# The prologue of an attention kernel with two MLPs shared out anew between the engines

## The reference

```
q, k, v: (4, 8, 768, 64)   mem_k, mem_v: (4, 8, 8, 64)   fp32
for each chunk of 32 queries:
    keys   = 8 memory keys + 16 to the left + the chunk + 8 to the right (clipped at the ends)
    scores = q_c @ keys.T / 8 ;  scores -= max(scores)
    a = exp(scores);  a /= sum(a) + 1e-9
    out_c = a @ values
x = out as (3072 tokens, 512)
h = x @ w_in (512 x 2048);  g = max(h, 0) + alpha * min(h, 0);  y = g @ w_out (2048 x 512)
z = (y @ w_a) * (y @ w_b) (512 x 1536);  result = z @ w_out2 (1536 x 512)
```

## Time and profile before

| | |
|---|---|
| median of 3 runs | 1223.64 us (1218.63, 1223.64, 1223.72) |
| profiled execution | 1219.24 us, span 1217.4 us |
| TensorE busy | 1205.3 us, 6634 matmuls |
| VectorE busy | 783.9 us (64%) |
| ScalarE busy | 571.8 us (47%) |
| GpSimd busy | 248.7 us (20%) |
| DMA | 87.84 MB, 72 GB/s on the mean |
| granted TensorE clock | 1.00 |

### The profile page before, as it was taken

One profiled execution on the slowest core, in us unless ns is written; L12 is line 12 of the kernel. 1 busy time (PEld: TensorE's weight loads), 2 busy tenths in 40 slices (PEclk: granted clock), 3 DMA queues, 4 the chain that ended last, 5 costly groups with the idle time before them and its releaser, 6 DMA issues.

```text
span 1217.4 us, 19013 instructions
## 1 busy us (share of the span) xinstructions
PE 1205.3 (99%) x6634; PEld 1095.9 (90%) x6637; DVE 783.9 (64%) x1452; ACT 571.8 (47%) x1412; POOL 248.7 (20%) x226
## 2 busy tenths in 40 slices
PE   8899999999999999999999999999999999999998
PEld 5799999999999999999999888888888888888887
DVE  7788777777777777777656466854376644465421
ACT  6765545454545455454323455543444443444322
POOL 1687323332323232323025100000000000000000
PEclk9999999999999999999999999999999999999999
DMA  6453212212112121121021411022102021111000
GB/s 268 134 154 112 85 60 72 71 58 84 58 58 84 58 84 58 58 85 40 5 92 35 160 74 70 36 96 69 44 35 70 35 97 68 44 36 69 1 36 34
DMA packets 27612, 87.84 MB, mean 72 GB/s; under 512 B 2720, under 2 KB 6816, under 8 KB 25248
## 3 DMA queue, kind: packets, MB, share of 16 engines
q1 hardware_dynamic: 23328, 80.76, 19.7%
q10 hardware_dynamic: 4224, 6.29, 1.4%
HBM read 74.46 MB, written 12.58 MB: 71 GB/s over the span
## 4 chain that ended last, share of the span: by engine, by line
PE 95%; DVE 3%; ACT 1%; issue 1%; POOL 0%; ACTq 0%; DVEq 0%; POOLq 0%
PE bank L570 15%; PE bank L572 15%; PE bank L571 15%; PE bank L578 9%; PE bank L577 9%; PE bank L576 9%; PE bank L813 5%; PE bank L814 5%; PE bank L812 5%; PE bank L620 2%; PE bank L589 1%; PE bank L588 1%; PE bank L595 1%; DVE g_lo L1206 0%; PE bank L605 0%
## 5 line engine op out<-in xcount | busy, mean ns | idle before, releaser
L577 PE MATMUL bank<-yc,ws 128*128 128x512 f32 x504 | 196.1, 389 | 0.0
L578 PE MATMUL bank<-yc,ws 128*128 128x512 f32 x504 | 196.1, 389 | 0.0
L576 PE MATMUL bank<-yc,ws 128*128 128x512 f32 x504 | 196.1, 389 | 0.0
L1196 DVE TENSOR_SCALAR g_neg<-bank,al 128x384 f32<-128x384 f32 x128 | 79.0, 617 | 121.2 <-PE bank L572 121.2
L883 ACT ACTIVATE prob<-prob,neg_max 96x128 f32<-96x128 f32 x220 | 85.7, 391 | 110.5 <-DVE neg_max L1161 110.5
L577 PEld LDWEIGHTS bank<-yc,ws 128*128 128x128 f32 x504 | 94.6, 188 | 19.7
L578 PEld LDWEIGHTS bank<-yc,ws 128*128 128x128 f32 x504 | 94.6, 188 | 19.6
L576 PEld LDWEIGHTS bank<-yc,ws 128*128 128x128 f32 x504 | 94.6, 188 | 19.6
L1392 DVE TENSOR_TENSOR p_split<-p_all,p_split 128x512 fp32r<-128x512 f32 x72 | 49.5, 691 | 93.5 <-ACT p_split L1078 93.4
L912 ACT ACTIVATE g_hi<-g_raw 128x384 fp32r<-128x384 f32 x128 | 67.1, 525 | 86.7 <-DVE g_raw L1201 84.1
L1078 ACT ACTIVATE p_split<-p_all 128x512 fp32r<-128x512 f32 x72 | 45.2, 631 | 110.3 <-PE bank L814 100.8
(11 more groups left out here) (150 smaller groups left out, 3036.8 us busy)
## 6 DMA issues: line engine op xcount, KB each, us to landing
u_raw<-units SPq DMA_DIRECT2D x53, 576.0 KB, 3.7
wr<-w_ab SPq DMA_DIRECT2D x18, 1024.0 KB, 4.8
u_early<-units SPq DMA_DIRECT2D x11, 576.0 KB, 8.8
y_dram<-y_stage ACTq DMA_DIRECT2D x8, 768.0 KB, 3.9
out<-o_stage SPq DMA_DIRECT2D x24, 256.0 KB, 2.0
w_raw<-w SPq DMA_DIRECT2D x16, 256.0 KB, 3.3
y_stage<-w SPq DMA_DIRECT2D x16, 256.0 KB, 3.0
wr<-y_dram SPq DMA_DIRECT2D x8, 512.0 KB, 4.4
```

Source lines behind the costliest of these rows:

```text
L576: nc.tensor.matmul(out_ap, w_hi, m_hi, start=first, stop=False, skip_group_check=True)
L577: nc.tensor.matmul(out_ap, w_hi, m_lo, start=False, stop=False, skip_group_check=True)
L578: return nc.tensor.matmul(out_ap, w_lo, m_hi, start=False, stop=True, skip_group_check=True)
L1196: nc.vector.tensor_scalar(g_neg[:, :], h_ps[:, 0:TOK], 0.0, al[:, j:j + 1], ALU.min, ALU.mult)\
```

## The change

In the prologue and in the tiles, `softmax_max` becomes four `tensor_tensor_reduce` operations per unit (one for each block): the sum of scores and mask, times -1/8 (or -1/16, see below), with the minimum of the result written out as the negated maximum; the exponential then has the scale -1. TensorE's next score waits for all four. `score_early` multiplies all 128 rows, in which k and q stand twice, so that early scores are twice as large and their scale is halved. The 1e-9 is added by a reduction over the sum and a constant beside it instead of by an operation with a scalar.

In the prologue GpSimd normalises instead of VectorE, and VectorE copies the transposes instead of ScalarE. The halves of a pair (mix, x_hi, x_lo) alternate, one for each unit, and unit 8's softmax stands in the loop with the others. The early weight pieces, v and k/q splits are placed anew. The fillers read a constant of ones that the program has anyway; there are ten ahead of the first score instead of eight, four to two for the first units, none for units 3 to 7 and fewer around tile 0. The last pair's mix is put one part of `up` later, `lo_g` of the first chunk ahead of the softmax. VectorE's loop over t = 1 to 5 is written out, since the mask of a block is now picked by a number.

```diff
+        def inverses(b):
+            return inv_sum[:, b].rearrange("p (b o) -> p b o", o=1).to_broadcast([QB, BLOCKS, KEYS])
+
+        def score_scale(u):
+
+            return -SCALE / 2 if u <= HEADS else -SCALE
...
         def w_in_prologue(u):
-            return {1: (0,), 2: (1,), 6: (2,), 8: (3,)}.get(u, ())
+            return {0: (0,), 2: (1,), 5: (2,), 8: (3,)}.get(u, ())
...
-            for n in range(W_PROLOGUE):
-                lo_w(n)
-            lo_v(HEADS, HEADS)
-            lo_unit(HEADS + 1, HEADS + 1)
+            def normalise(u):
+                buf = prob_early[u % 2]
+                pool.wait_ge(inv_done, u + 1)
+                nc.gpsimd.tensor_tensor(buf[:, :, :], buf[:, :, :], inverses(u % 2), ALU.mult).then_inc(prob_done, 1)
+
+            for u in range(HEADS + 1):
+                normalise(u)
+                for n in w_in_prologue(u):
+                    lo_w(n)
+                if u == 4:
+                    lo_v(HEADS, HEADS)
+                if u == 6:
+                    lo_v(HEADS + 1, HEADS + 1)
+            pool.wait_ge(w_lo_done, W_PROLOGUE)
+            pool.wait_ge(v_lo_done, 2)
+            lo_kq(HEADS + 1, HEADS + 1)
...
                 if not isinstance(u, int) or u >= 1:
-                    pe.wait_ge(mask_added, u)
+                    pe.wait_ge(neg_done, u)
...
             def keep_busy(n):
 
+                ones = nc.const_aps.tensor(1.0, [P, 512], mybir.dt.bfloat16)
                 for i in range(n):
-                    nc.tensor.matmul(o_ps[:, :], filler[:, 0:P], filler[:, P:], start=True, stop=True)
+                    nc.tensor.matmul(o_ps[:, :], ones[:, 0:P], ones, start=True, stop=True)
 
             def score_early(u):
 
                 pe.wait_ge(early_loaded[u], 16)
                 if u:
-                    pe.wait_ge(mask_added, u)
+                    pe.wait_ge(neg_done, u)
                 for i in range(BLOCKS):
-                    q = u_early[0:HEAD_DIM, u, Q0 + i * QB:Q0 + (i + 1) * QB]
+                    q = u_early[:, u, Q0 + i * QB:Q0 + (i + 1) * QB]
                     at = slice(i * KEYS, (i + 1) * KEYS)
-                    last = nc.tensor.matmul(s_ps[0:QB, at], q, u_early[0:HEAD_DIM, u, at], start=True, stop=True)
+                    last = nc.tensor.matmul(s_ps[0:QB, at], q, u_early[:, u, at], start=True, stop=True)
...
                 for kt in range(KT):
-                    if first_tile and j == 0 and kt == 1:
-
+                    if first_tile and j == 0 and kt == 2:
+                        keep_busy(2)
                         mix_early(PAIRS - 1, 0)
                         mix_early(PAIRS - 1, 1)
...
-                            if first and j == 1:
-                                keep_busy(3)
...
                             if first and p == 0:
-                                keep_busy(4)
+                                keep_busy(2)
...
-            pe.wait_ge(filler_ready, 1)
-            keep_busy(8)
+            keep_busy(10)
             score_early(0)
             for u in range(HEADS + 1):
-                keep_busy(3)
+                if u < 3:
+                    keep_busy(4 - u)
                 if u < HEADS:
                     score_early(u + 1)
-                if u >= 3 and u % 2:
-                    mix_early(u // 2 - 1, 0)
-                    mix_early(u // 2 - 1, 1)
-                if u in (1, 2, HEADS):
-                    keep_busy(3)
                 if u == 1:
                     pe.wait_ge(consts, 1)
                 if u:
-                    transpose_probs(u - 1, u % 2 == 1)
+                    if u < 3 or u == HEADS:
+                        keep_busy(3)
+                    transpose_probs(u - 1, False)
+                if u >= 3 and u // 2 <= PAIRS:
+
+                    mix_early((u - 3) // 2, (u - 3) % 2)
...
                     last = nc.scalar.activation(dst[:, i, :], src[:, i, :], ACT.Exp,
-                                                bias=neg_max[:, b, i:i + 1], scale=SCALE,
-                                                accum_out=row_sum[:, b, i:i + 1])
+                                                bias=neg_max[:, b, i:i + 1], scale=-1.0,
+                                                accum_out=row_sum[:, b, i, 0:1])
...
-            def copy_pt(u):
-
-                act.wait_ge(transposed, u + 1)
+            for u in range(HEADS + 1):
+                exps(u, u % 2, masked_early[u % 2], prob_early[u % 2])
                 if u >= 4:
-                    act.wait_ge(mixed, u - u % 2 - 2)
-                nc.scalar.activation(pt_early[:, (u // 2) % 2, :, u % 2, :],
-                                     pt_ps[:, 0:TOK].rearrange("p (b q) -> p b q", b=BLOCKS),
-                                     ACT.Copy).then_inc(pt_copied, 1)
-
-
-            for u in range(HEADS):
-                exps(u, u % 2, masked_early[u % 2], prob_early[u % 2])
-                if u >= 3 and u % 2:
-                    split_x(u // 2 - 1, 0, u // 2 - 1, 0, True)
-                    split_x(u // 2 - 1, 1, u // 2 - 1, 0, True)
-                if u:
-                    copy_pt(u - 1)
+                    split_x((u - 4) // 2, u % 2, (u - 4) // 2, 0, True)
                 for n in w_in_prologue(u):
                     hi_w(n)
+                if u == 3:
+                    hi_v(HEADS, HEADS)
                 if u == 5:
-                    hi_v(HEADS, HEADS)
-                if u == 6:
                     hi_v(HEADS + 1, HEADS + 1)
-            copy_pt(HEADS - 1)
-            for n in w_in_prologue(HEADS):
-                hi_w(n)
-            hi_kq(HEADS + 1, HEADS + 1, 0)
+                if u == 7:
+                    hi_kq(HEADS + 1, HEADS + 1, 0)
+            split_x(PAIRS - 2, 1, PAIRS - 2, 0, True)
             split_x(PAIRS - 1, 0, PAIRS - 1, 0, True)
             split_x(PAIRS - 1, 1, PAIRS - 1, 0, True)
-            exps(HEADS, 0, masked_early[0], prob_early[0])
...
-                nc.vector.tensor_tensor(dst[:, :, :], s_ps[0:QB, :].rearrange("p (b k) -> p b k", b=BLOCKS),
-                                        mask[:, bass.ds(half, BLOCKS), :], ALU.add).then_inc(mask_added, 1)
-                dve.wait_ge(mask_added, u + 1)
-                nc.vector.tensor_reduce(row_max[:, b], dst[:, :, :], AX_X, ALU.max).then_inc(max_done, 1)
-                dve.wait_ge(max_done, u + 1)
-                nc.vector.tensor_scalar(neg_max[:, b], row_max[:, b], -SCALE, None, ALU.mult)\
-                    .then_inc(neg_done, 1)
-
-            def normalise(u, b, buf=prob):
+
+                for i in range(BLOCKS):
+                    last = nc.vector.tensor_tensor_reduce(
+                        out=dst[:, i, :], in0=s_ps[0:QB, i * KEYS:(i + 1) * KEYS], in1=mask[:, half + i, :],
+                        scale=score_scale(u), scalar=FAR, op0=ALU.add, op1=ALU.min, accum_out=neg_max[:, b, i:i + 1])
+                last.then_inc(neg_done, 1)
+
+            def invert_sums(u, b):
                 dve.wait_ge(exp_done, u + 1)
-                nc.vector.tensor_scalar(row_max[:, b], row_sum[:, b], 1e-9, None, ALU.add).then_inc(sum_done, 1)
+                nc.vector.tensor_reduce(row_total[:, b], row_sum[:, b], AX_X, ALU.add).then_inc(sum_done, 1)
                 dve.wait_ge(sum_done, u + 1)
-                nc.vector.reciprocal(inv_sum[:, :], row_max[:, b]).then_inc(inv_done, 1)
+                if isinstance(u, int) and u >= 2:
+                    dve.wait_ge(prob_done, u - 1)
+                nc.vector.reciprocal(inv_sum[:, b], row_total[:, b]).then_inc(inv_done, 1)
+
+            def normalise(u, b):
+                invert_sums(u, b)
                 dve.wait_ge(inv_done, u + 1)
-                nc.vector.tensor_tensor(buf[:, :, :], buf[:, :, :],
-                                        inv_sum[:, :].rearrange("p (b o) -> p b o", o=1)
-                                        .to_broadcast([QB, BLOCKS, KEYS]),
-                                        ALU.mult).then_inc(prob_done, 1)
+                nc.vector.tensor_tensor(prob[:, :, :], prob[:, :, :], inverses(b), ALU.mult).then_inc(prob_done, 1)
+
+            def copy_pt(u):
+                dve.wait_ge(transposed, u + 1)
+                if u >= 4:
+                    dve.wait_ge(mixed, u - u % 2 - 2)
+                nc.vector.tensor_copy(pt_early[:, (u // 2) % 2, :, u % 2, :],
+                                      pt_ps[:, 0:TOK].rearrange("p (b q) -> p b q", b=BLOCKS)).then_inc(pt_copied, 1)
...
                     bend(t, 4 * p, first)
                     if attention:
                         split_pt(g * 2, 0)
+                    if first and p == 0:
+                        lo_g(t, 0)
+                    if attention:
                         softmax_max(g * 2 + 1, 1, half, prob)
-                    lo_g(t, 4 * p)
+                    if not (first and p == 0):
+                        lo_g(t, 4 * p)
                     if p == 0 and not first:
...
+            nc.vector.memset(row_sum[:, :, :, 1], 1e-9)
...
```

(27 more changed lines are left out.)

16 lines of the change are left out of this document (5 added, 11 removed).

## The result

The changed kernel takes 1212.75 us (median of five runs, 1212.38 to 1214.58) against 1219.34 for the kernel before, run beside it (five runs, 1218.63 to 1223.72): a ratio of 0.9937 with an interval of 0.9914 to 0.996. The direction held, and 1212.75 lies in the range, 0.75 us from its lower end. The size didn't hold: profiled execution against profiled execution the forecast was 3.9 us, and it is 6.9 (1212.38 against 1219.24; spans 1210.6 and 1217.4). Nor did the likeliest outcome: I gave 0.57 to a change of under 6.1 us and 0.35 to a larger gain, and the medians are 6.6 us apart.

A forecast was written before the change was run, and what follows sets the result against it. TensorE was taken to bound the kernel, with VectorE setting T8 in the prologue. Gains of 0.6 + 0.2 + 1.3 + 1.8 = 3.9 us took the median of 1223.64 to 1219.7 us, range 1212 to 1226.

The forecast's parts named there:

- The price s: VectorE time of a unit's four fused softmax operations: 1.5 us, between 1.2 and 1.95, in place of 1.54.
- high bound: Each fused softmax operation pays an accumulator read as long as ScalarE's, 0.19 us, which makes s 1.95 us.
- T8: Time when TensorE begins unit 8's transposes: 40.0 us against 40.62, 0.6 gained, with ends of +3.3 and -3.4.
- formula: Prologue: first softmax at 6.8, five periods of s + 1.2, three of s + 1.7, then the tail: T8 = 26.5 + 9s.
- the units are in before they are needed: Prologue DMAs keep their order, and 418 GB/s from 10 to 20 us fall to 58 after 30, so data comes in time.
- The start: Before the first score: an earlier filler start can bring the clock up sooner, 0 to 0.65 us, 0.2 taken.
- Pair 1: Fillers ahead of TensorE's wait for g_lo go and g_lo moves ahead of the softmax: 1.3 us gained.
- Pairs 3 and 4: The sum on VectorE, now a reduction, takes 0.17 instead of 1.07 us: 0.9 off each pair, 1.8 together.
- A: Rival: fused operation cheap (s = 1.2), tile 0 gets back what it can; 7.1 to 9.3 us gained, 1214.3 to 1216.5; chance 0.28.
- B: Rival: fused operation pays its accumulator read in full (s = 1.95); 3.4 lost, 3.3 gained, 1223.7 us; chance 0.20.
- C: Rival: with fewer prologue fillers TensorE's clock falls; 9.8 us lost, 3.7 gained, 1229.7; chance 0.10.
- D: Rival: busy GpSimd hands the gain back as waits for weights; about 1 us gained, 1222.6; chance 0.07.

The follow-up runs named there:

- e10_two_moved: The changed kernel with two ScalarE steps one unit later, the high part of v of unit 8 and the third weight piece: 1210.75 us.
- e12_last_weight_later: `e10_two_moved` with the fourth weight piece split later, behind the last x_hi on ScalarE and behind lo_kq of unit 9 on GpSimd: 1209.56 us.
- e2_fused_one_by_one: The changed kernel with a wait between the four fused softmax operations of a unit, so each starts when the one before has ended: 1212.29 us.
- e6_g_lo_behind: The changed kernel with g_lo of the first chunk behind the softmax again: 1212.48 us.
- e1_three_ops: The changed kernel with the softmax as three operations again (mask added, maximum, negated maximum), in prologue and tiles: 1216.63 us.
- f1_fused_alone: The kernel before with only the four fused softmax operations, TensorE's wait for them and VectorE's loop written out: 1214.99 us.
- e7_scalar_sum: The changed kernel with the sum of a unit in the tiles as an operation with a scalar again instead of a reduction: 1214.20 us.

## Why the prediction was right or wrong, step by step

**The price s: the step that failed.** I had 1.5 between 1.2 and 1.95; it is 0.93. The length was right (0.283 for 0.29), the distance between starts was not: I took it to be the length, a small gap and 0.08 for the read of the accumulator, 0.38 in all, and it is 0.213. The high bound, an accumulator read paid in full, fell as well: the read takes 0.08 and lies under the next operation. One of my two rows, the x_lo pieces of the earlier trace rows, does start as far apart as it is long (0.36 and 0.352). Another row of the same trace showed that this isn't general:

```profile
10.68 0.69 DVE L1170 TENSOR_TENSOR prob<-prob,inv_sum 96x512 f32<-96x512 f32 x1
11.29 0.68 DVE L1156 TENSOR_TENSOR y_stage<-bank,mask 96x512 f32<-96x512 f32 x1
```

The second starts 0.61 us after the first, which is 0.69 long. The x_lo pieces alternate between the lower and the upper 64 partitions; these two and the fused operations all start at partition 0. The Trainium skill (VectorE: DVE Perf Modes, Two Vector instructions with no wait between them) says that an instruction is held until the earlier ones end when an input or its output starts in another quadrant than the last one read from, or written to, the same memory. The spacings, 0.21 for the ones and 0.36 for the others, agree with it; no run here changed the quadrants alone, so that the form of the operations makes the difference isn't excluded. The Trainium skill (VectorE: DVE Perf Modes, The DRAIN you can't avoid) tells of chained copies that took the same time with and without waits, and adds that an operation that isn't held starts earlier. Here it does: 0.21 apart without a wait, 0.33 with one. The mere number of operations, which had spoken for the high bound, does not decide here: four fused ones take 0.93 us where three took 1.54.

I also priced the negated maximum of the kernel before at the 0.17 of an undisturbed stretch. In its prologue it takes 0.353 on the mean:

```profile
L1161 DVE TENSOR_SCALAR neg_max<-row_max 96x4 f32<-96x4 f32 x9 | 3.2, 353 | 0.3
```

**T8.** The formula's sum comes close where ScalarE waits for no DMA (33.9 and 33.8 for the measured 34.24 and 33.80 of `e10_two_moved` and `e12_last_weight_later`), but in part by luck. In `e10_two_moved` the first five periods take 11.5 us instead of 5(s + 1.2) = 10.7, the next three 7.0 instead of 3(s + 1.7) = 7.9, and the tail 9.05 instead of 8.6. VectorE's period from unit 5 on is s + 1.4, because the reciprocal and the copy too are overlapped by what follows them:

```profile
19.58 0.29 DVE L1157 CUSTOM_DVE_ANT_0 y_stage<-bank,mask 96x128 f32<-96x128 f32 x1
...
20.43 0.15 DVE L1164 TENSOR_REDUCE row_total<-row_sum 96x4 f32<-96x8 f32 x1
20.62 0.17 DVE L1168 RECIPROCAL inv_sum<-row_total 96x4 f32<-96x4 f32 x1
20.71 0.54 DVE L1179 COPY pt_early<-bank 128x384 f32<-128x384 f32 x1
21.17 0.71 DVE L1193 TENSOR_TENSOR x_lo<-bank,x_hi 64x192 fp32r<-64x192 f32 x2
21.91 0.29 DVE L1157 CUSTOM_DVE_ANT_0 y_stage<-bank,mask 96x128 f32<-96x128 f32 x1
```

In `e2_fused_one_by_one`, with s = 1.28, the formula gives 37.9 and is 0.9 too high. ScalarE's 2.2 us a unit left out what else it does: with `hi_v` (0.40), a weight piece (0.63) or `hi_kq` (0.95) between, its exponentials of units 5 to 8 start 2.7, 2.9 and 3.2 us apart in `e10_two_moved`. The changed kernel falls short of the formula by 2.0 us, and the sentence that failed there is that the units are in before they are needed. I checked that against the mean bandwidth of the kernel before and not against the new place of `hi_v(8)`: two units earlier in a faster loop, it came up at 15.9 us and its data at 18.05. In the kernel before it ran at 25.51, without a wait. Which share the new place has and which the faster loop wasn't taken apart; with the two steps moved T8 comes 2.35 us earlier. That GpSimd takes 1.3 for the normalisation was too much (1.03), the copy's length of 0.55 right (0.534), the score of full height as assumed 1.08.

**The start.** 0.2 forecast, 0.28 measured (6.81 to 6.53), but between kernels with the same start it lies anywhere from 5.74 to 7.08, mostly by when the higher clock comes: the ten fillers take 3.75 to 4.43 us, and the score behind them 1.04 to 1.91. It is chance more than a gain.

**Pair 1.** 1.3 forecast, 0.94 measured, for a reason that was half wrong: the order of g_lo gives nothing (`e6_g_lo_behind`), while the fused softmax gives it (1.44 lost in `e1_three_ops`; 0.81 gained in `f1_fused_alone`, which keeps the fillers). It takes out the negated maximum of 1.24 us, about 1.1 of it excess, that I had not seen ahead of g_lo.

**Pairs 3 and 4.** 0.9 each forecast and 0.89 and 0.92 measured, but the cause I gave isn't needed for it. Without the reduction (`e7_scalar_sum`) they take 20.7 us all the same, and so they do with the fused softmax alone (20.66 and 20.69 in `f1_fused_alone`), or with the reduction and no fused softmax (20.75 and 20.81 in `e1_three_ops`, which keeps every other part of the change). Either seems to shift VectorE against GpSimd enough to miss the collision; that wasn't shown by itself. What the reduction does buy is certainty, 1.4 us in pair 2 of `e7_scalar_sum`. Pair 5 lost 0.35; there g_lo waits for ScalarE's g_hi, and which edit does it stays open.

**The rivals.** A, the cheap operation, was the right mechanism with too high a price: it gave 1214.3 to 1216.5, and the median came out below. It did so by the base alone; as a gain A had 7.1 to 9.3 us, and 6.6 to 6.9 came. B fell with s. C didn't come in the changed kernel, but it is near: 0.72 behind a wait of 3.3 us and 0.50 without fillers are two small edits away. D fell: among TensorE's waits is none for weights any more. GpSimd does show as its longest wait, in the prologue, yet it mostly hands on ScalarE's delay.

**The base.** I set the steps against a median of 1223.64, which lies on the upper of the two levels. Against the profiled run the same steps read 1215.3. I widened the range by the 5 us between the runs; they are two levels 4.7 us apart, and in the one trace of the upper level that there is, a slow start goes with it. That the range held owes more to this width than to the steps.

**The signs.** Pairs 3 and 4 at 20.7, the clock of 1.00, no wait for g_lo in pair 1 and 20.17 us for the undisturbed pairs came as I had named them. The scores 2.7 us apart (2.2), the fused operations 0.38 apart (0.21) and T8 at 40.0 (36.59) did not.

## What to carry to other kernels

Price a new operation by its length and by the distance between starts, each from a row of its own: a distance read off instructions that alternate between halves of the partitions is not the cost of ones that don't. When a loop gets faster than its bound, or a step is moved forward in it, look for the next bound on every queue, the steps that wait for a DMA in the middle of another engine's loop first; here two such steps, which the change had moved forward, were worth as much as the regrouping when they went back by one unit each. Read the duration of a small operation in the stretch that is to be changed, not in a quiet one. And undo one part at a time before crediting any: pairs 3 and 4 gained just what was forecast, and would have without the edit I credited.

## What was not expected of the hardware

- A VectorE operation of 0.283 us can start 0.21 us after its like; a wait between the two puts the start 0.12 us later.
- TensorE's first stretch at 1.2 GHz is over by the end of the first score (5.6 to 6.9 us) in 13 of the 14 traces, but lasts to about 17 us in the profiled run of `f1_fused_alone`, and the clock's column shows 1.00 in both. The 4.7 us between the two levels of that kernel probably hang on it.
- Whether VectorE is held beside GpSimd depends on the form: 96x4 as an operation with a scalar took 0.15 to 1.24 us, as a reduction 0.14 to 0.16.
